# Rows for the gate logits turned on VectorE instead of TensorE, the logits on 64x32 tiles, the keys in a ring of four, and parts of the weight splits on GpSimd

## The reference

```python
# x [8, 8, 512, 64], state [8, 8, 32, 64]
scores = scale * x @ state.T ; a = softmax(scores) ; xread = a @ state
scores2 = scale * state @ x.T ; a2 = softmax(scores2) ; sread = a2 @ x
rows = concat([xread, sread], tokens) -> [8 * 544, 512]
h = rows @ w_in                         # 512 x 2048
y = (h * clip(h + 3, 0, 6) / 6) @ w_out
logits = y @ w_gate                     # 512 x 8
e = argmax(logits) ; gate_w = softmax(logits)[e]
eom = sigmoid(y @ w_output_gate)        # 512 x 8
out = gate_w * eom[e] * (relu(y @ w1[e]) @ w2[e])   # w1 512 x 1024, w2 1024 x 512
```

## Time and profile before

| | us |
|---|---|
| median of 3 runs (1128.51 to 1131.19) | 1130.11 |
| the profiled execution | 1128.17 |
| its span | 1126.4 |
| PE busy | 1104.0 (98%) |
| DVE busy | 658.5 (58%) |
| ACT busy | 476.6 (42%) |
| POOL busy | 74.7 (7%) |

### The profile page before, as it was taken

How to read it: one execution, slowest core, us unless ns; L and a number is a source line. 1 busy time by engine, 2 the same in 40 slices (tenths; PEclk the granted TensorE clock), 3 DMA queues, 4 the chain that set the end, 5 groups by cost and what they waited for, 6 DMA issues and landing times.

```text
span 1126.4 us, 20220 instructions
## 1 busy us (share of the span) xinstructions
PE 1104.0 (98%) x6199; PEld 872.0 (77%) x6200; DVE 658.5 (58%) x1269; ACT 476.6 (42%) x789; POOL 74.7 (7%) x95
## 2 busy tenths in 40 slices
PE   9999999999999999999999999899999999999996
PEld 7777777777777777777777988677888888878885
DVE  6674665655655646646555455875665645558632
ACT  4454434434443443444354445343444333435320
POOL 0000100100101001001001010100011110101011
PEclk9999999999999999999999999999999999999999
DMA  9210211111102102111004079659877654785541
GB/s 364 106 39 1 76 39 38 38 39 38 43 33 75 38 1 76 38 38 40 1 1 132 1 260 285 197 174 284 263 240 232 218 173 139 234 258 181 168 154 60
DMA packets 129794, 135.59 MB, mean 120 GB/s; under 512 B 13999, under 2 KB 107823, under 8 KB 127152
## 3 DMA queue, kind: packets, MB, share of 16 engines
q1 hardware_dynamic: 95056, 87.26, 24.9%
q10 hardware_dynamic: 28896, 29.36, 8.3%
q0 software_dynamic: 5760, 17.90, 4.3%
HBM read 90.06 MB, written 45.47 MB: 120 GB/s over the span
## 4 chain that ended last, share of the span: by engine, by line
PE 87%; DVE 5%; DMA 2%; ACT 2%; issue 2%; SPq 1%; ACTq 1%; DVEq 0%; POOL 0%; POOLq 0%
PE y_ps L964 34%; PE h_ps L946 16%; PE y_ps L1038 15%; PE h_ps L1014 7%; PE y_ps L1014 6%; PE a_ps L921 3%; PE h_ps L936 2%; DMA hid_mv<-hidden 1%; DVE we L564 1%; ACT we L1210 1%; PE a_ps L819 1%; PE a_ps L905 1%; SPq L663 1%; PE a_ps L885 1%; PE b_ps L827 1%
## 5 line engine op out<-in xcount | busy, mean ns | idle before, releaser
L964 PE MATMUL y_ps<-w_out_hi,hid_hi 128*128 128x512 f32 x512 | 204.7, 400 | 0.0
L964 PE MATMUL y_ps<-w_out_hi,hid_lo 128*128 128x512 f32 x512 | 199.7, 390 | 0.0
L964 PE MATMUL y_ps<-w_out_lo,hid_hi 128*128 128x512 f32 x512 | 199.4, 389 | 0.0
L1038 PE MATMUL y_ps<-we,act_t_hi 128*128 (+1 forms) x608 | 188.5, 391 | 4.2 <-DVE yo L1616 2.2
L946 PE MATMUL h_ps<-att_hi,mix 128*128 128x512 f32 x512 | 184.1, 402 | 0.1
L1550 DVE SCALAR_TENSOR_TENSOR hid<-hid,h_ps 128x512 f32<-128x512 f32 x128 | 87.7, 685 | 144.9 <-ACT hid L1159 144.9
L1159 ACT ACTIVATE hid<-h_ps,three 128x512 f32<-128x512 f32 x128 | 87.9, 687 | 150.5 <-PE h_ps L946 150.4
L1038 PEld LDWEIGHTS y_ps<-we,act_t_hi 128*128 128x128 f32 x608 | 114.6, 189 | 28.9 <-issue 5.3
L964 PEld LDWEIGHTS y_ps<-w_out_hi,hid_hi 128*128 128x128 f32 x512 | 96.0, 188 | 49.1 <-issue 30.4
L1558 DVE TENSOR_TENSOR hid_lo<-hid,hid_hi 128x512 fp32r<-128x512 f32 x128 | 88.0, 687 | 62.8 <-ACT hid_hi L1166 62.3
L1038 PE MATMUL y_ps<-we,act_t_lo 128*128 (+1 forms) x304 | 118.7, 391 | 0.0
(11 more groups left out here) (251 smaller groups left out, 1511.7 us busy)
## 6 DMA issues: line engine op xcount, KB each, us to landing
raw<-in_w ACTq DMA_DIRECT2D x12, 2048.0 KB, 10.6
hid_mv<-hidden SPq DMA_DIRECT2D x148, 128.0 KB
hidden<-expert_hid SPq DMA_DIRECT2D x70, 256.0 KB
xg<-buckets SPq DMA_DIRECT2D x156, 64.0 KB
xb<-in_x_rows SPq DMA_DIRECT2D x8, 1024.0 KB, 4.8
x_t<-in_x_t SPq DMA_DIRECT2D x7, 1024.0 KB, 4.9
buckets<-pad_row SPq DMA_DIRECT2D x8, 774.0 KB, 8.0
w_in_raw<-in_w_in SPq DMA_DIRECT2D x4, 1024.0 KB, 13.5
```

The costliest lines, as they stand in the source:

```text
L964: i = pe.matmul(y_ps[:, t, :], hid_of(b, j)[1 + hp][:, t * P:(t + 1) * P], w_out_s[wp][:, j, :], start=(j == 0 and m == 0), stop=(j == KF ...
L1038: i = pe.matmul(y2_ps[:, slot % 2, :], act_t[hp][:, slot % 2, f, :], we[:, bass.ds(w_at + (wp * WPART + KD * F + f * DM), DM)], start=(f = ...
```

## The change

- The steps `T4` and `T` are gone. In their place a step `X` n is done by VectorE: a stream transpose of one row tile, which turns each 32x32 block in place, into `rows_x`.
- `L4` takes such rows. It is 32 products on 64x32 tiles of the array: for each 128 columns c, each 32-row part, and each half g of 64 partitions (which hold two 32-token strips), weights of 64x32 from a new table `wg` that holds the gate columns twice, once for each strip, with zeros between. The half g goes to bank g, so `L4` needs both banks. ScalarE copies each bank out, duplicated into the layout that `LT` turns; VectorE then reduces in four parts of 32 partitions instead of once.
- The last 512 rows and the states use the same `X`, `L4`, `LT` instead of `T`, `L`.
- The keys lie in one tile of four blocks; those of blocks 4 to 7 are loaded one at a time when a place is free. Small tensors and `hid_s` move in memory.
- Around the table, GpSimd takes pieces 2 and 3 of the second expert's w1 low parts and all four of its w2; `wait`s for `w1_lo_pool` are added on TensorE and SyncE. ScalarE splits the star's w2 in two halves around the first ReLU, and loads the second expert's w2 later, behind the ReLUs of tile 2. Two small table steps come earlier.

```diff
@@ -117,12 +117,16 @@
-    keys_s = [at("keys0", o, [P, half_b, PAIRS, NS], F32)]
+    keys_s = at("keys", o, [P, half_b, PAIRS, NS], F32)
...
-    rows4_t = at("rows4_t", o, [P, KD, S], F32)
-    logits_t = at("logits_t", o, [P, S], F32)
+    rows_xs = [at("rows_x", o, [P, CH, DM], F32), at("rows_x_last", 147456, [P, CH, DM], F32),
+               at("rows_x_state", 131072 + 8192, [P, ST, DM], F32)]
...
-    POST_LAST = {0: [("T", 0)], 2: [("L", 0), ("T", 1)], 4: [("L", 1), ("T", 2)], 6: [("L", 2), ("T", 3)],
-                 8: [("L", 3)], 12: [("R", 0)], 16: [("C", 0)]}
-    POST_STATE = {0: [("T", 0)], 1: [("L", 0), ("T", 1)], 2: [("L", 1)], 4: [("R", 0)]}
-    POST = {2: [("T4", 0), ("T4", 1)], 5: [("T4", 2), ("T4", 3)], 7: [("L4", 0)], 9: [("LT", 0)], 13: [("R", 0)]}
+    POST = {2: [("X", 0)], 4: [("X", 1), ("X", 2)], 5: [("X", 3)], 7: [("L4", 0)], 9: [("LT", 0)], 13: [("R", 0)]}
+    POST_LAST = {0: [("X", 0)], 2: [("X", 1), ("X", 2)], 4: [("X", 3)], 6: [("L4", 0)], 8: [("LT", 0)], 12: [("R", 0)],
+                 16: [("C", 0)]}
+    POST_STATE = {0: [("X", 0), ("X", 1)], 1: [("L4", 0)], 2: [("LT", 0)], 4: [("R", 0)]}
...
@@ SyncE @@
             if b >= 1 and b + 1 < B and ("LT", 0) in post_steps(b, half):
                 load_values(b + 1)
+                if half_b <= b + 2 < B:
+                    wait(sp, "m_ps", MIXES * (b + 3 - half_b))
+                    sp.dma_start(keys_of(b + 2), keys[b + 2]).then_inc(sem("keys_loaded1"), 16)
...
-        sp.dma_start(keys_s[1][:], keys[half_b:B].rearrange("b p q m -> p b q m")).then_inc(sem("keys_loaded1"), 16)
...
+            if is_b(t.n, 1):
+                sp.wait_ge(sem("lt_ps"), B + 1)
...
         sp.wait_ge(sem("w1_ready"), 2)
+        sp.wait_ge(sem("w1_lo_pool"), 1)
@@ GpSimd @@
+        split_lo(pool, 0, 1, WSLOT, (2, 3), "w1_lo_pool")
         scatter_rows(B, ST)
...
-        for n in range(PRE):
-            body(Tile(0, n))
+        body(Tile(0, 0))
+        split_lo(pool, 1, 1, WSLOT, (0, 1, 2))
+        body(Tile(0, 1))
+        split_lo(pool, 1, 1, WSLOT, (3,), "w2_ready")
+        body(Tile(0, 2))
@@ TensorE @@
-                if name in ("T", "T4"):
-                    wait(pe, "y_out_act" if n < 2 else "y_out_dve", 2 * pb + n % 2 + 1)
-                    for c in range(KD):
-                        i = pe.transpose(bank_ap(k)[:, c * P:(c + 1) * P], rows_of(pb)[:, n, c * P:(c + 1) * P], ident[:])
-                    i.then_inc(sem("t_ps"), 1)
-                elif name == "L4":
+                if name == "X":
+                    continue
+                tiles = tiles_in(pb)
+                if name == "L4":
...
-                    wait(pe, "rows_t_ready", CH * (pb + 1))
-                    for c in range(KD):
-                        i = pe.matmul(bank_ap(k)[4 * E * c:4 * E * c + 4 * E, :], wg[:, c, :], rows4_t[:, c, :],
-                                      start=True, stop=True)
+                    wait(pe, "rows_x_ready", CH * pb + tiles)
+                    for g in range(2):
+                        for free in bank_free(b, half, g):
+                            wait(pe, *free)
+                    for c in range(DM // P):
+                        for part in range(P // NS):
+                            for g in range(2):
+                                i = pe.matmul(bank_ap(g)[NS * part:NS * part + NS, 0:NS * tiles],
+                                              wg[2 * NS * g:2 * NS * g + 2 * NS, 4 * c + part, :],
+                                              rows_x_of(pb)[2 * NS * g:2 * NS * g + 2 * NS, :,
+                                                            P * c + NS * part:P * c + NS * part + NS],
+                                              start=(c == 0), stop=(c == DM // P - 1))
...
-                elif name == "L":
-                    wait(pe, "rows_t_ready", CH * pb + n + 1)
-                    for c in range(KD):
-                        i = pe.matmul(bank_ap(k)[:, 0:2 * E], rows_t_of(pb)[:, c, :], wg[:, c, 0:2 * E],
-                                      start=(c == 0), stop=(c == KD - 1))
...
+            if is_b(t.n, PRE):
+                pe.wait_ge(sem("w1_lo_pool"), 1)
@@ ScalarE @@
-                    act.activation(logits_t[:], bank_ap(BANK_OF[name, n]), ACT.Copy
-                                   ).then_inc(sem("logits_t_ready"), 1)
+                    for g in range(2):
+                        act.activation(logits_t_of(pb)[:].rearrange("p (t g u i) -> p t g u i", t=tiles, g=2, u=2)[:, :, g],
+                                       bank_ap(g)[:, 0:NS * tiles].rearrange("p (t i) -> p t i", t=tiles).unsqueeze(2)
+                                       .to_broadcast([P, tiles, 2, NS]), ACT.Copy).then_inc(sem("logits_t_ready"), 1)
...
-        side(B + 1, 0)
+        split_hi(1, 0, 0, (0, 1))
         relu(Tile(0, 0), 0)
-        split_hi(1, 0, 0)
-        act.dma_start(by_pieces(raw2_first[1]), w2[0].rearrange("i p c -> p i c")).then_inc(sem("raw2_loaded"), 16)
+        split_hi(1, 0, 0, (2, 3))
         relu(Tile(0, 0), 1)
         side(B + 1, 1)
         rows_hi(Tile(0, 2))
         split_hi(0, 1, WSLOT, (0, 1))
         relu(Tile(0, 1), 0)
         side(B + 1, 2)
+        relu(Tile(0, 1), 1)
         split_hi(0, 1, WSLOT, (2, 3))
-        relu(Tile(0, 1), 1)
         hidden_hi(Tile(0, 0))
         relu(Tile(0, 2), 0)
         relu(Tile(0, 2), 1)
+        act.dma_start(by_pieces(raw2_first[1]), w2[0].rearrange("i p c -> p i c")).then_inc(sem("raw2_loaded"), 16)
         hidden_hi(Tile(0, 1))
-        split_hi(1, 1, WSLOT)
         hidden_hi(Tile(0, 2))
+        split_hi(1, 1, WSLOT, (0, 1))
         rows_hi(Tile(0, 3))
+        split_hi(1, 1, WSLOT, (2, 3))
         rows_hi(Tile(0, 4))
@@ VectorE @@
+                if name == "X":
...
+                    if not (is_b(pb, B - 1) or is_b(pb, B)):
+                        wait(dve, "sr_ps", b + 1)
+                    dve.transpose(rows_x_of(pb)[:, n, :], rows_of(pb)[:, n, 0:DM]).then_inc(sem("rows_x_ready"), 1)
                 elif name == "LT":
                     wait(dve, "lt_ps", pb + 1)
-                    dve.tensor_reduce(logits[:], bank_ap(BANK_OF[name, n]).rearrange(
-                        "p (t c e) -> p t e c", t=CH, c=KD)[:, :, 0:2 * E, :], AX.X, ALU.add
+                    for q in range(P // NS):
+                        own = slice(NS * q, NS * q + NS)
+                        dve.tensor_reduce(logits[own, 0:tiles, :], bank_ap(BANK_OF[name, n])[own, 0:P * tiles].rearrange(
+                            "p (t c u e) -> p t u e c", t=tiles, c=KD, u=2)[:, :, q % 2], AX.X, ALU.add
...
         mlp_block(B, NSB, ST)
+        dve.wait_ge(sem("iota2"), 5)
+        chain(dve.tensor_scalar(upto[:], upto[:], 0.0, None, ALU.is_ge))
+        chain(dve.memset(t_chg[:, MT - 1:MT], 0.0))
+        side(B + 1, 0)
         split_lo(dve, 1, 0, 0, signal="w2_ready")
         turn_rows(Tile(0, 2))
-        side(B + 1, 1)
         rows_lo(Tile(0, 2))
-        split_lo(dve, 0, 1, WSLOT, (0, 1))
         side(B + 1, 2)
-        split_lo(dve, 0, 1, WSLOT, (2, 3), "w1_ready")
+        split_lo(dve, 0, 1, WSLOT, (0, 1), "w1_ready")
         turn_hidden(Tile(0, 0))
...
-            if is_b(t.n, PRE):
-                split_lo(dve, 1, 1, WSLOT, signal="w2_ready")
```

134 lines of the change are left out of this document (63 added, 71 removed).

## The result

The changed kernel takes 1139.59 us (median of 6 runs, 1136.35 to 1141.28) against 1130.36 us before (6 runs, 1128.51 to 1131.49): ratio 1.0083, 95% interval 1.0067 to 1.0100. It is slower by 9.2 us; 1115.3 was predicted, with 1108 to 1125 as the range. The prediction is wrong in sign. The profiled execution of the changed kernel took 1141.28 us, the longest of the six, so its span is 13.1 us above before's where the medians are 9.2 apart. Beside the experiments the kernel before took 1129.9 to 1130.0 us, 0.4 less than here; "less than after" can be too large by that much.

The account below looks back on a forecast made before the run. It took TensorE, busy 98% of the span, to bound the kernel: 9.8 (middle blocks) + 0.3 (state block) + 4.7 (tail) = 14.8 us off 1128.17, with 1.94 added for the runs' median 1115.3 us; range 1108 to 1125.

Parts of the forecast that it names:

- TensorE's saving: Middle blocks: two T4 pairs leave TensorE, 1.74 us a block; the logits product takes 1.03 us, 0.04 more than before.
- The 0.3 us that came back: Middle blocks: without T4 in front, the first hidden slice's second-layer product waits for its low part, 0.3 us a block.
- The first rival: Logits product serialises by row half, 1.9 instead of 1.03 us, 6.3 us back in seven blocks, 1121.6 us; chance 0.12.
- The cover holds: Middle blocks: VectorE's added transposes and reductions, 4.0 us a block, stay hidden; otherwise the cost is under 1 us a block.
- 9.8 forecast: Seven middle blocks together: 1.40 us gained in each, 9.8 us in all, bounds 3.5 to 12.6.
- State block: VectorE's choice, for which TensorE waits, begins 0.3 us earlier; gain 0.3 us, bounds 0 to 3.4.
- Second layer of tile 0 4.1 us earlier: Start of the star expert: tile 0's second layer starts at about 704.3 instead of 708.46, 4.1 us earlier.
- Tile 2's chain ends near 717.3, wait 2.0: Experts: with the moved load beside it, tile 2's chain ends near 717.3; TensorE, there at 715.2, waits 2.0 us.
- the second rival: GpSimd's six pieces hold up VectorE's two-input steps around the experts' start; 7.1 us saved, 1123.0 us; chance 0.28.
- hidden at 2.4: Experts: at 2.4 us a piece, all six of GpSimd's weight pieces end before they are wanted.
- The clock: At 705 to 710 us no fall to 1.2 GHz is expected with one wait of 1.3 us; 1.2 us comes back.
- tail 4.7: Expert tiles: tile 3 starts 4.7 us earlier, booked as the tail's gain, bounds 0 to 8.

Follow-up runs that it names:

- e4: The changed kernel with one mix product, the one behind the logits' transposes, half a slice later: 1133.89 us, ratio to before 1.0035.
- r11: Changed kernel with GpSimd's subtractions on VectorE, load back early, mix product later, and the choice's exponentials ahead of tile 1's first ReLU: 1123.88 us.
- r12: As r11, and besides two first-layer weight pieces on VectorE moved behind tile 0's low parts: 1122.19 us, ratio to before 0.9943.
- e2: The changed kernel with only the load of the second weights moved back to its earlier place; GpSimd's pieces stay: 1134.69 us, ratio to before 1.0045.
- e8: The kernel before with only the load of the second weights issued behind tile 2's ReLU: 1135.91 us, ratio to before 1.0053.
- e1: The changed kernel with GpSimd's six subtractions back on VectorE; the moved load stays: 1130.55 us, ratio to before 1.0006.
- e3: The changed kernel with both GpSimd's six subtractions back on VectorE and the load at its earlier place: 1126.49 us, ratio to before 0.9971.
- e7: The kernel before with only the six subtractions of the second expert's weights moved to GpSimd: 1138.73 us, ratio to before 1.0080.
- r10: Changed kernel with load back early, mix product later, and only the two first-layer pieces on GpSimd, whole: 1122.27 us, ratio to before 0.9938.

## Why the prediction was wrong

Against the profiled execution it forecast a span of 1126.4 - 14.8 = 1111.6 us; it was 1139.5, 27.9 more (the medians are 24.3 apart).

- **TensorE's saving: right.** T4's 1.74 us went, and the logits group takes 1.09 us (1.03). The 0.3 us that came back was right in size by luck: not the first second-layer product waits, as forecast, but slice 2's first, for slice 0's clip to leave its half of `h_ps`. The first rival, a logits group of 1.9 us, falls.
- **"The cover holds": failed.** I held the three added reductions (1.3 us) only against slice 5, which waits for VectorE. The one that waits for the reductions themselves is the next writer of the bank that they read. That user comes six products behind the transposes, at 192.29 if it had not to wait, and the reductions run from 191.10 to 192.88. Cost: 0.64 us a block, 4.5 us in seven; e4 got back 3.9. Most of the 5.0 us between 9.8 forecast and 4.8 measured.
- **State block: the path right, the clock left out.** 0.3 gained forecast, 0.4 lost in the profiled execution. The choice began 12.0 us behind the block's first product instead of 12.7, and the product that waits for it was 0.57 us nearer (0.3 forecast). But TensorE now waits 1.83 us there instead of 0.40, and in this execution the clock fell behind it, which took 1.0 us; in the executions without the fall the block gained 0.6.
- **"Second layer of tile 0 4.1 us earlier": failed, 0.3 earlier.** Three terms. ScalarE and VectorE did start earlier: VectorE's low parts of w2 begin at 686.00, 3.9 us behind the first expert product instead of 5.4, so 1.5 instead of 3.5. The two pieces given to GpSimd saved 2.36 us and stretched the other two by 2.2. The four reductions take 1.23 us (forecast 1.0); the rest, in ScalarE's waits and the last steps, no run took apart. The earliest start of any version is r11's, 21.70, 1.6 us nearer than before; in r12 VectorE already waits for the hidden values themselves.
- **"Tile 2's chain ends near 717.3, wait 2.0": mis-sized.** The collision was seen, but the sum gave it no price: the ReLU's end at 704 and the chain of 14.0 us make 718.0 without any load beside it, already more than 717.3. Measured, the write under the 2 MB load takes 11.2 us to the reading back instead of 4.9, and TensorE waits 4.7. e2 gives 4.9 us back; in the kernel before the same move costs 5.9 (e8).
- **GpSimd: the second rival was the case.** The piece's price was right (2.4 forecast, 2.35 to 2.40), and so was "hidden at 2.4"; the blocking was given a chance of 0.28 and 7.7 us. It costs 9.0 us here (e1), 8.2 with the load early (e2 against e3) and 8.7 in the kernel before (e7). In the sum it was booked at nothing because no row of before had both engines at work, but that was no evidence against it. The rival's own result, 1123.0, was still 16.6 us too low, since it took the other two causes for gains.
- **The clock: mis-sized.** I expected no fall. The changed kernel's stretch 705 to 710 us stands at 0.50 of 2.4 GHz, against 0.79, behind TensorE's waits of 3.75 and 1.11 us:

```profile
700.00:705.00 5.00, 0.24 (x2) 0.10 (x1) 4.83 (x12) 2.19 (x4) 3.74 (x2) 0.84 0.57 149
705.00:710.00 5.00, 4.90 (x12) 3.88 (x13) 4.66 (x12) 1.22 (x2) 1.79 (x2) 0.50 0.98 300
```

In the changed kernel the clock stood at 1.2 GHz for 6.8 us around and behind these two waits and for 3.4 us each at those of 4.7, 3.2, 2.3 and 1.9 us and at the state block's of 1.83; before had one stretch of 3.4 us in all these places. So a wait can cost more than its own length, 1.6 us more for tile 6's second layer. It need not: the wait of 3.1 us ahead of tile 6 in r10 had no fall behind it, and the same wait of 1.83 us had one in some executions and none in others.

In sum: blocks 5.0, state block 0.7, tail 4.7 + 14.1 = 18.8, behind it 2.1, and 1.3 of a later start (the blocks gained 4.8 and the state block lost 0.4, but the first expert product is only 3.1 earlier; 1.1 of it shows already in block 0, whose first second-layer product is at 24.34 instead of 23.24): 27.9 us. Not tested are the 3.3 us by which e3 still reaches tile 6 later than before: 1.3 of them are between tile 0's second layer and tile 3 and 2.2 behind tile 3 (0.25 were gained ahead of both). The traces place most of them: tile 0's second layer takes 7.92 us instead of 6.86, with the clock at 1.2 GHz for 6.8 us instead of 3.4, and two waits behind tile 3 are 2.06 and 2.99 us instead of 1.05 and 2.19. No run tests why.

## What to carry to other kernels

Work given to GpSimd beside a chain of short VectorE steps is not free even if each piece is hidden by its own due time: price it as up to one GpSimd instruction for each VectorE step with SBUF inputs that it can meet, and put it where VectorE is idle or reduces. When an instruction is split in several, look at who next writes what they read, not only at who waits for the engine. A large load that is moved to a quiet place on its own queue should be held against each small transfer of a dependent chain in its 10 us; here such a chain went through memory, and the load cost 5 to 6 us.
